# One program text per engine in each branch, or a branch that is left and rejoined: attention, soft mixture and top-1 mixture in one launch

## The reference, cut to what matters

```python
scores = q @ k.T / 8 + bias            # 4 x 8 heads, 768 tokens, head size 64; first 8 keys and last 96 kept
attn = softmax(scores) @ v             # -> x, 3072 tokens of 512 features
logits = x @ phi                       # 32 slots, 4 for each of 8 experts
slot_in = softmax(logits, axis=0).T @ x
slot_out[e] = relu(slot_in[e] @ w1[e]) @ w2[e]
x = softmax(logits, axis=1) @ slot_out
e = argmax(x @ w_gate)                 # second mixture: one expert for each token
out = gate * (relu(x @ v1[e]) @ v2[e])
```

## Time and profile before

| | us |
|---|---|
| median of 3 runs | 441.06 |
| the three runs | 438.9, 441.06, 441.35 |
| the profiled execution | 438.9 |
| its span | 437.1 |
| outside the span | 1.8 |
| PE busy | 420.4 (96% of the span) |
| DVE busy | 239.6 |
| ACT busy | 212.3 |
| POOL busy | 210.1 |

### The profile page before, as it was taken

How to read it: one execution, slowest core, us unless ns; L and a number is a source line. 1 busy time by engine, 2 the same in 40 slices (tenths; PEclk the granted TensorE clock), 3 DMA queues, 4 the chain that set the end, 5 groups by cost and what they waited for, 6 DMA issues and landing times.

```text
span 437.1 us, 9388 instructions
## 1 busy us (share of the span) xinstructions
PE 420.4 (96%) x3024; PEld 351.8 (80%) x3025; DVE 239.6 (55%) x791; ACT 212.3 (49%) x418; POOL 210.1 (48%) x216
## 2 busy tenths in 40 slices
PE   8999999999999999998979989999999999999994
PEld 7899999999999998553326967778888888888883
DVE  6667777767767775557101778483333333233344
ACT  3888788788888773322010025473233333333333
POOL 4999999999999910010001021244333333444430
PEclk9999999999999999999998999999999999999999
DMA  7856989889977379379996469311111111112110
GB/s 230 288 222 253 406 347 394 342 352 349 374 249 239 113 251 390 146 265 377 381 387 204 115 262 374 128 60 60 60 54 54 48 48 60 60 60 60 36 54 12
DMA packets 29173, 89.21 MB, mean 204 GB/s; under 512 B 3440, under 2 KB 6000, under 8 KB 29136
## 3 DMA queue, kind: packets, MB, share of 16 engines
q1 hardware_dynamic: 25456, 78.47, 48.6%
q0 software_dynamic: 3360, 9.83, 7.3%
q10 hardware_dynamic: 320, 0.42, 0.4%
HBM read 80.85 MB, written 8.13 MB: 204 GB/s over the span
## 4 chain that ended last, share of the span: by engine, by line
PE 80%; DMA 9%; POOL 4%; DVE 3%; issue 1%; ACT 1%; SPq 0%; ACTq 0%; DVEq 0%; POOLq 0%
PE O L466 16%; PE Yq L1640 11%; PE Yq L1641 10%; PE Yq L1642 10%; PE PT L448 8%; DMA ext<-in_moe_w 5%; PE S L439 5%; PE S L438 4%; PE Gp L1571 3%; PE XTp L914 3%; DMA w2h<-in_moe_w 2%; PE Cp L1543 2%; PE Up L923 1%; PE Lp L1003 1%; POOL kl L401 1%
## 5 line engine op out<-in xcount | busy, mean ns | idle before, releaser
L543 ACT ACTIVATE shared<-shared,nm 128x256 f32<-128x256 f32 (+1 forms) x192 | 83.7, 484 | 29.7 <-DVE nm L656 29.6
L466 PE MATMUL O<-V,PTs 128*128 128x65 f32 x704 | 90.1, 269 | 0.0
L656 DVE CUSTOM_DVE_ANT_0 shared<-S,TA 128x256 f32<-128x256 f32 (+1 forms) x192 | 68.8, 396 | 34.5 <-PE S L439 32.4
L466 PEld LDWEIGHTS O<-V,PTs 128*128 128x128 f32 x704 | 86.5, 191 | 1.2 <-issue 1.0
L1640 PE MATMUL Yq<-w2h,hh 128*128 x208 | 83.0, 399 | 0.4 <-issue 0.4
L1641 PE MATMUL Yq<-w2l,hh 128*128 x208 | 81.2, 390 | 0.0
L1642 PE MATMUL Yq<-w2h,hl 128*128 x208 | 81.1, 390 | 0.0
L1940 DVE SCALAR_TENSOR_TENSOR hl<-Gp,hh 128x512 fp32r<-128x512 f32 x56 | 38.2, 689 | 39.9 <-ACT hh L1752 37.8
L401 POOL TENSOR_TENSOR kl<-k_raw,kh 128x816 fp32r<-128x816 f32 x30 | 57.9, 1931 | 3.9 <-ACT kh L558 1.7
L397 POOL TENSOR_TENSOR qs<-q_raw,qs 64x768 fp32r<-64x768 f32 x30 | 54.8, 1827 | 2.4
L448 PE MATMUL PT<-ident,shared 128*128 128x128 f32 x352 | 54.9, 275 | 0.0
(11 more groups left out here) (248 smaller groups left out, 568.5 us busy)
## 6 DMA issues: line engine op xcount, KB each, us to landing
mem<-in_moe_w SPq DMA_DIRECT2D x9, 2048.0 KB, 11.2
ext<-in_moe_w SPq DMA_DIRECT2D x6, 2048.0 KB, 15.4
V<-in_v SPq DMA_DIRECT2D x16, 715.0 KB, 6.7
k_raw<-in_k SPq DMA_DIRECT2D x13, 816.0 KB, 6.8
q_raw<-in_q SPq DMA_DIRECT2D x13, 768.0 KB, 4.5
xmem<-in_moe_w SPq DMA_DIRECT2D x2, 2048.0 KB, 8.4
w2h<-in_moe_w SPq DMA_DIRECT2D x1, 2048.0 KB
w2l<-in_moe_w SPq DMA_DIRECT2D x1, 2048.0 KB, 15.9
```

Source lines behind the costliest of these rows:

```text
L466: mm = pe.matmul(O[grp % 2][:, at:at + VC], PTs[:, par, (h * kbs + kb) * P:(h * kbs + kb + 1) * P], V[buf][:, h, vb, :], start=(n == 0), s ...
L543: nc.scalar.activation(Pb[:, par, h, 0:width(g)], Pb[:, par, h, 0:width(g)], ACT.Exp, bias=nm[:, par, h:h + 1], scale=-1.0).then_inc(exp_d ...
L656: v.tensor_tensor_reduce(Pb[:, par, h, 0:w], S[par][h][:, 0:w], tab, -SCALE, HUGE, ALU.add, ALU.min, nm[:, par, h:h + 1]).then_inc(biased, 1)
```

## The change

The closures go, and PE and DVE rejoin after a branch as the other engines do.

- On PE the `If` holds the attention and `front()` (up to the end of `experts(0)`) in both branches. `experts(1)`, the end of the soft mixture and all of `top1_moe` stand once, behind the `Else`. At the end of `front()` PE now branches over `general()` and the second copy of `front()`.
- On DVE the `If` holds the attention's 96 steps without the last group's `sums`, `invert`, `norm`. Behind the `Else` a second `If` on the same flag holds these three, and then the soft and top-1 stages follow once. After the last step DVE now branches over `general()`.
- At the program's end no copy stands between the last instruction of either engine and the end block.
- No matmul, vector instruction, transfer or semaphore operation of the taken path is added or removed. SP, ACT and POOL keep their instructions.

```diff
-    def attend_dve(dve):
+    @block.vector
+    def _(dve):
...
-        def usual():
+        n0 = n[0]
+        with dve.If(fast > 0):
...
                 if g % GT == 2 and grp >= 0:
                     norm(grp)
-            sums(GROUPS - 1)
-            invert(GROUPS - 1)
-            norm(GROUPS - 1)
-
-        def general():
+        with dve.Else():
+            n[0] = n0
...
             dve.sem_inc(attended, GROUPS)
-        return fast, usual, general
+        with dve.If(fast > 0):
+            sums(GROUPS - 1)
+            invert(GROUPS - 1)
+            norm(GROUPS - 1)
...
-        front()
+        begin, usual, general = attend(pe)
+        fast = begin()
+        with pe.If(fast > 0):
+            usual()
+            front()
+        with pe.Else():
+            general()
+            front()
         for grp in range(1, EG):
             experts(grp)
...
-    @block.tensor
-    def _(pe):
-        begin, usual, general = attend_pe(pe)
-        fast = begin()
-        with pe.If(fast > 0):
-            usual()
-            soft_pe(pe)
-            route_pe(pe)
-        with pe.Else():
-            general()
-            soft_pe(pe)
-            route_pe(pe)
...
-    @block.vector
-    def _(dve):
-        fast, usual, general = attend_dve(dve)
-        with dve.If(fast > 0):
-            usual()
-            soft_dve(dve)
-            route_dve(dve)
-        with dve.Else():
-            general()
-            soft_dve(dve)
-            route_dve(dve)
```

More of the change, by code:

```diff
@@ L126, in build @@
         attended = sem("attended")
-        attend_pe, attend_dve = attention(nc, ctx, sb, psum, sem, block, attended, mem, ext, X, shared, ident, ones, Rsel, phi_sb, wg_sb, load_piece,
+        attend = attention(nc, ctx, sb, psum, sem, block, attended, mem, ext, X, shared, ident, ones, Rsel, phi_sb, wg_sb, load_piece,
                   sp_passed, const_ready, rsel_ready, small_loaded, q_d, k_d, v_d, n_d, phi_d, wg_d)
-        soft_pe, soft_dve = soft_moe(nc, ctx, sb, psum, sem, block, attended, mem, ext, xmem, X, ident, ones, Rsel, phi_sb, load_piece,
+        soft_moe(nc, ctx, sb, psum, sem, block, attend, attended, mem, ext, xmem, X, ident, ones, Rsel, phi_sb, load_piece,
                  slot_loaded, rsel_ready, small_loaded, STR, Cn, CT, c_stored, st_out, ct_out, counting, r_iota, lt_done, c_dram)
         xst.close()
-        top1_moe(nc, ctx, sb, psum, sem, block, attend_pe, attend_dve, soft_pe, soft_dve, sp_passed, ident, ones, Rsel, wg_sb, mem, STR, CT, counting,
+        top1_moe(nc, ctx, sb, psum, sem, block, sp_passed, ident, ones, Rsel, wg_sb, mem, STR, CT, counting,
                  c_stored, st_out, ct_out, r_iota, lt_done, v1_d, v2_d, c_dram, out_d)
@@ L759, in general, with soft_moe @@
             dve.sem_inc(attended, GROUPS)
-        return fast, usual, general
+        with dve.If(fast > 0):
+            sums(GROUPS - 1)
+            invert(GROUPS - 1)
+            norm(GROUPS - 1)
     st.close()
-    return attend_pe, attend_dve
-def soft_moe(nc, ctx, sb, psum, sem, block, attended, mem, ext, xmem, X, ident, ones, Rsel, phi_sb, load_piece,
+    return attend
+def soft_moe(nc, ctx, sb, psum, sem, block, attend, attended, mem, ext, xmem, X, ident, ones, Rsel, phi_sb, load_piece,
              slot_loaded, rsel_ready, small_loaded, STR, Cn, CT, c_stored, st_out, ct_out, counting, r_iota, lt_done, c_dram):
@@ L899, in _ @@
                        C4.rearrange("p t r s -> p t (r s)")).then_inc(c_stored, 16)
-    def soft_pe(pe):
+    @block.tensor
+    def _(pe):
         def turn(k, q):
@@ L1122, in _ @@
         nc.scalar.copy(y_parts, Yp).then_inc(y_out, 1)
-    def soft_dve(dve):
+    @block.vector
+    def _(dve):
         v = nc.vector
@@ L1235, in soft_moe, with top1_moe @@
     st.close()
-    return soft_pe, soft_dve
-def top1_moe(nc, ctx, sb, psum, sem, block, attend_pe, attend_dve, soft_pe, soft_dve, sp_passed, ident, ones, Rsel, wg_sb, mem, STR, CT, counting,
+def top1_moe(nc, ctx, sb, psum, sem, block, sp_passed, ident, ones, Rsel, wg_sb, mem, STR, CT, counting,
              c_stored, st_out, ct_out, r_iota, lt_done, v1_d, v2_d, c_dram, out_d):
@@ L1537, in _ @@
         pool.sem_inc(pool_step, 1)
-    def route_pe(pe):
+    @block.tensor
+    def _(pe):
         def busy(count):
@@ L1829, in _ @@
             rank_done(rank, first + units)
-    def route_dve(dve):
+    @block.vector
+    def _(dve):
         v = nc.vector
```

5 lines of the change are left out of this document (3 added, 2 removed).

## The result

| | before | changed |
|---|---|---|
| median of 10 runs, us | 439.99 | 444.50 |
| range, us | 438.9 to 441.8 | 442.55 to 446.2 |
| the profiled execution | 438.9 | 445.38 |
| its span | 437.1 | 443.7 |

The ratio is 1.0092, with a 95% interval of 1.0066 to 1.0117: **slower by 4.5 us**, 0.9%. The range of the prediction (439.2 to 446.5) holds it, the likeliest case (442.4, within 0.5% of before) doesn't.

A forecast was written before the change was run, and what follows sets the result against it. PE, busy 96% of the span, was taken to bound the kernel, with far branches deciding the change. Terms -0.8 (end), +2.1 (DVE's branch) and 0 (PE's branch) gave +1.3 on 441.06: 442.4 us, range 439.2 to 446.5.

The forecast's parts named there:

- The end of the program: Kernel's end: without DVE's branch, POOL's drain, ending at 436.1, is next to be late; span ends 0.8 us earlier.
- rival D: Kernel's end: POOL's drain shrinks too (-2.3) and DVE's branch is covered; 438.8 us, faster; chance 0.05.
- DVE's branch: End of attention, behind norm of group 30: sums starts 2.3 us late (1.0 to 2.6), costing +2.1 us.
- the cover of 2 us: At DVE's new branch: sums waited for PE until 168.32 anyway, which covers 2.0 us from 166.3.
- the wait of PE for the copy after the fourth group: PE's turns of X: the fifth group waits for DVE's first copy, so PE stops for 2.1 us.
- the 1.9 us from fetch to resume: DVE's branch: the next instruction comes 1.9 us after the program fetch starts, as at the kernel's end before.
- PE's branch: Between the groups of experts: 3.9 us, array 0.9 us late, covered by the 3.03 us wait for piece 14; cost 0.
- Rival B: PE's branch between expert groups outlasts its cover; 444.3 to 446.3 us, slower; decided by a resume past 217 us; chance 0.15.
- Does the delay reach the end?: From DVE's branch onward: the chain stays on PE and transfers don't buy time back, so +2.1 us reaches the end.
- A: DVE's branch is cheap, its target held or landed by 168.3; only the end's gain of -0.8 remains, 440.3 us; chance 0.18.
- C: PE's unit loop: a block edge inside makes branches back cost up to 3.9 us; 448 to 485 us, slower; chance 0.12.
- the margin of 0.2 us: PE's turns: DVE's first copy was done at 169.9, the fifth group due at 170.1, so 0.2 us of delay is absorbed.

The follow-up runs named there:

- dve_only: The changed kernel with PE as in the kernel before, so only DVE rejoins; 445.05 us, ratio 1.0096 to the kernel before.
- dve_late: The kernel before with PE unchanged and DVE rejoining behind the experts' second relu, where it waited 15.4 us; 439.70 us, ratio 0.9991 to before.
- pe_only: The kernel before with only the PE part of the change, DVE's branch at the end kept; 439.85 us, ratio 0.9993 to before.
- inside: The changed kernel with the last group's sums, invert and norm inside the If, ahead of DVE's branch; 439.16 us, ratio 0.9980 to before.

## Why the prediction was right in its range and wrong in its sum

**The end of the program (-0.8 predicted, -2.2 in the trace).** The term was mis-sized. DVE was through with its drain within 0.1 us of its last instruction's end (443.4), in substance as said. POOL's drain did not shrink (rival D's words); it started earlier, because the last store landed 1.4 us sooner. I took 431.4 as fixed, since no row tied it to DVE. It is tied to PE: where PE keeps its branch (`dve_only`, `dve_late`), POOL's drain is next in line and the gain is 0.6 to 0.8 us, as predicted.

**DVE's branch (+2.1 predicted; 5.3 to 5.4 in the trace, 5.7 to 6.0 by medians).** This is the step that failed. The place, the cover of 2 us, the wait of PE for the copy after the fourth group, and the 1.9 us from fetch to resume all came out. Two things were wrong in it. First, the start of the fetch. I read "a fetch starts only at 168.8 to 169.0 in this load" as a time by which DVE's piece would have come; it is a start whose request the trace doesn't show. The wait counts from the request: 3.8 us behind a branch under load, so 166.6 + 3.8 = 170.4 and `sums` 3.9 us late, not 2.6 at most. The upper bound was a bound on nothing. Second, the sum had no term for PE's clock behind a stop, 1.5 us here; the 16 products of 2.42 us behind the 3.03 us stop in the earlier trace rows were a sign of it.

**PE's branch (0 predicted; -0.4 by medians in `pe_only`, not clear of noise, and 0.2 us late at the slots' output).** The size was wrong, 6.6 to 6.8 us instead of 3.9, with two fetches in it where the end has one, and the stretch after it ran at half clock, and still nothing shows: the DMA-bound stretch reaches to the last piece at 234.8. Rival B's border, a resume past 217 us, was passed (217.2 in `pe_only`), and its price did not come: "up to 3.0 us is covered" was too little.

**Does the delay reach the end?** Yes, as predicted; the transfers gave nothing back (`dve_only`: 7.1 us at 197 and at 237).

**The rivals.** A (cheap branches, 440.3) is false for this change and true with a nearer target: 438.50 to 438.75. It stood or fell with where an edge between fetched pieces lies, which could have been asked of the distance (196 instructions against pieces of some 126). C (a loop over an edge) is false: PE's loop branch keeps its price, its rounds are (423.2 - 302.0) / 10 = 12.1 us, and no fetch of PE's text lies in between:

```profile
L1703 PEldq COMPARE_BRANCH  x11: 76/207/241, 302.0 to 423.2; - x11
```

D had the end right and DVE wrong. The slowdown of 0.9% had a chance of 0.33 and came by the path that I had called likeliest at less than half its size, not by B or C. That the range holds 444.50 is luck: its upper part was put there for B. The likeliest time looks closer (442.4, 2.1 us short) than the likeliest change was (+1.3 against +4.5, 3.2 us short), because the three runs that it started from had a median of 441.06, 1.1 us above that of all ten (439.99).

Two edges of the prediction don't follow from its own terms: with the margin of 0.2 us taken off at both ends the forecast's range ends at 442.7, not 442.9, and C starts at 441.06 + 1.3 + 6.6 = 449, not 448. Neither changes the reading.

## What to carry to other kernels

Behind the attention's last step, with DMA at about 400 GB/s, DVE's branch over code that isn't run cost 0.2 to 0.6 us when it reached up to 118 instructions ahead, and 5.6 us or more from 162 on; so make the skipped path short (a loop instead of copies gave 6.0 us here), or rejoin where the engine has some 7 us of waiting to spare. Price such a branch by the DMA load at its place, counted from the branch, and allow for the matrix engine's half clock if it will stand behind it. A copy of the program behind the last instruction costs at the end, and an engine off the critical path may make its neighbours late there, through its fetches as far as these traces tell.

## What the runs showed of the hardware that I had not expected

- A fetch of DVE's text started 1.0 to 1.3 us behind the branch with DMA idle, 3.8 us at about 400 GB/s, and 4.9 us behind a store that kept all DMA engines busy at 283 GB/s. From there to the next instruction it was 1.8 to 2.0 us.
- The price is a step between 112 and 162 instructions (0.5 us, 5.6 us), and three instructions' difference in the place of the branch changed it from 5.8 to 2.1 us.
- PE's branch in the middle of the program took 6.0 to 6.9 us in nine traces, with the resume 2.4 to 3.0 us behind the second of two fetches; at the end it took 3.7 to 4.0 us in four, 2.3 us behind a single one.
- The wait for the last store to land ended 1.8 us behind POOL's loop in ten traces without, and 3.0 to 3.4 us in four traces with, PE's branch over its copy.
- Behind PE's stops at the two branches in the changed kernel, `dve_only` and `pe_only` (3.4 to 3.8 us) the granted clock was 0.50 for 3.4 or 6.8 us, so a stop of 3.8 us cost 5.3. It stayed at 1.00 behind one of 3.75 us in `dve_late` and one of 1.6 us in `inside`.
